# Rows of x by VectorE's 32x32 transposition, gathered in quarters; 8-column logits on TensorE; q's decay on GpSimd; most of w3 loaded behind attention

## The chip, the core and the metric

The kernel runs on one core of a Trainium2 chip, in fp32 and in pairs of fp32r matrices. The metric is the device time of one execution in microseconds (us); lower is better. The engines work in parallel, each from its own instruction stream, and wait for each other on semaphores: TensorE (PE in the profile; its weight loads are PEld), VectorE (DVE), ScalarE (ACT), GpSimd (POOL) and SyncE (SP), which here only starts DMAs.

## The reference

Decayed linear attention feeds a mixture of experts with one expert per token, and that feeds a bilinear network:

```python
# B=4, H=8, S=768, D=64: state (64x64) per head
state = gamma * state + outer(k[t], v[t]);  y[t] = scale * q[t] @ state
x = y, as [3072 tokens, 512]
logits = x @ w_gate + modality_bias[modality_id]        # 8 experts
e = argmax(logits);  gate = softmax(logits)[e]
x = gate * (relu(x @ w1[e]) @ w2[e])                    # w1: 512x1024, w2: 1024x512
out = (((x @ wa) * (x @ wb)) @ w3) @ w_out              # d_ff = 1024
```

## The kernel before

**Attention** runs in 24 units u = 4c + b: six chunks c of 128 tokens, and in each the four batches b. TensorE computes for a unit the scores k q (line 744, into banks 2 and 3), the part that comes from the state (`from_state`, line 762), the part within the chunk (`from_chunk`, line 771) into banks 4 and 5, and the update of the state (`update`, line 783), which the last chunk leaves out. The result is x transposed, features in partitions. ScalarE copies it to `xTu` (four copies, line 553). `rows_and_logits` (line 754) of the unit before then multiplies each of the four 128x128 blocks of `xTu` by `iw`, which is an identity beside the gate weights, so 136 columns: 128 columns give the rows of x, 8 give logits, both in the PSUM pair of banks 6 and 7. VectorE adds up the logits (line 978), ScalarE copies the rows to `x_keep`, and SyncE stores them to `x_rows` in DRAM. VectorE also masks the scores (`prob`, lines 971 and 972), multiplies q by its decay (`qdk`, line 982) and writes the new state (line 990); GpSimd multiplies k by its decay (`kdk`, line 500). SyncE's queue loads q, k (two layouts) and v of a unit, 256 KB each, as soon as the unit four before has updated its state (`s_up`); behind them it stores the rows of five units before and brings in 256 KB of w_out (units 4 to 11) or of w3 (from unit 12 on, two in units 20 to 23). All of x, 24 tiles of 128 tokens, lies in DRAM when attention ends.

**Between attention and the experts** TensorE forms w3 @ w_out in eight products of 24 matmuls each (`w3_product`, line 382). Between them stand the last `rows_and_logits`, `counts` (lines 820 and 821), `token_of_place` (line 884) and, behind the first 6 matmuls of product 7, `first_x` (line 832), which transposes the first gathered window. Meanwhile one long chain of small VectorE operations chooses the experts, sorts the tokens and writes the tables of the windows. `tile_meta` (line 1132) gives GpSimd the list of tokens.

**The experts** run in 8 windows of up to four tiles (in this run 4, 3, 3, 3, 4, 4, 4 and 2 tiles: 512, 384 or 256 columns). `gather` on GpSimd makes the rows of a window with one indirect DMA per tile (line 517, four in a window), 128 rows of 2 KB each, and writes `meta_sorted`. It starts for window w when TensorE has transposed window w-1 (`s_ixp`). TensorE transposes window w+1 in the middle of window w. Its loop over windows has three bodies in the code, for 2, 3 and 4 tiles, in this order; two tests (lines 868 and 870, 871) lead to the right one. SyncE loads the experts' weights, 2 MB for w1 and 2 MB for w2 of each, when the copies in use have been split. The **bilinear part** behind the windows is TensorE's alone and isn't touched.

Of the kernel before, what the change touches and what calls it, by code (L numbers as in the profile page):

```python
# [30 lines left out]
def build(nc, q_t, k_t, k, v, mod_id, w_gate, mod_bias, we1, we2, wa, wb, w3_t, w_out, out):  # L31
# [18 lines left out]
    RANKED = 4  # L50
    XCH = 16
# [19 lines left out]
    def const(name, a):  # L71
# [4 lines left out]
    c_ident = const("c_ident", np.eye(P))  # L76
# [6 lines left out]
                ("token", S * (np.arange(NT) % B) + P * (np.arange(NT) // B) + pos[:, None])]  # L83
# [6 lines left out]
    x_rows = nc.dram_tensor("x_rows", [NT * P, DM], F32).ap()  # L90
# [4 lines left out]
    with ctx:  # L95
# [19 lines left out]
        XW = P + E  # L115
        iw = fixed("iw", [P, KD, XW])
# [3 lines left out]
        tile_meta = fixed("tile_meta", [P, 2, NX])  # L120
        x_id = fixed("x_id", [P, GT], I32)
# [26 lines left out]
        xTu = r("xTu", [P, KD, P])  # L148
# [90 lines left out]
        s_lg = sem("s_lg")  # L239
# [149 lines left out]
        def _(sp):  # L389
# [20 lines left out]
            def x_store(c, b, u):  # L410
                sp.wait_ge(s_keep, u + 1)
                sp.dma_start(x_rows[b * S + c * P:b * S + (c + 1) * P, :], x_keep[:, u, :]).then_inc(s_xst, 16)

            def sp_unit(c, b, u):
# [32 lines left out]
            sp.wait_ge(s_lg, NT)  # L447
# [41 lines left out]
        def _(pool):  # L489
# [13 lines left out]
            each_unit(kdecay)  # L503


            def gather(w):
# [6 lines left out]
                of_window = lambda a: a[:, :, bass.ds(tile, GT)] if w else a[:, :, 0:GT]  # L513
                pool.tensor_copy(x_id[:, :], of_window(tile_meta)[:, 0:1, :].rearrange("p a t -> p (a t)")).then_inc(s_xid, 1)
# [4 lines left out]
                pool.tensor_copy(win_meta[:, :, :], of_window(tile_meta).rearrange("p a t -> p t a")).then_inc(s_wmeta, 1)  # L519
# [17 lines left out]
            pool.tensor_copy(row_id[:, :], meta_in[:, :, 0:1].rearrange("p n a -> p (n a)")).then_inc(s_rowid, 1)  # L537
# [10 lines left out]
        def _(act):  # L548
            act.dma_start(qkv[:, 0, KT, :], slot_v[KT][0, 0, :, :]).then_inc(s_ldq[0], 16)
            act.dma_start(small[:, :], c_small).then_inc(s_const, 16)  # L550
            act.dma_start(iw[:, :, 0:P], c_ident.unsqueeze(1).to_broadcast([P, KD, P])).then_inc(s_gatew, 16)
            act.dma_start(iw[:, :, P:XW], w_gate.rearrange("(c p) e -> p c e", p=P)).then_inc(s_gatew, 16)
            copy = lambda o, i, **kw: act.activation(o, i, ACT.Copy, **kw)  # L553

            def keep(u):

                act.wait_ge(s_lg, u + 1)
                dst = x_keep[:, u, :]
                copy(dst.rearrange("p (j t) -> p j t", j=KD), pair[:, :, 0:P]).then_inc(s_keep, 1)
# [14 lines left out]
            def unit(c, b, u):  # L574

                if u:
                    keep(u - 1)
                act.wait_ge(s_yTu, u + 1)
                for odd in range(2):
                    for r in range(2):  # L580
                        rows = slice((r ^ odd) * D, (r ^ odd) * D + D)
                        i = copy(xTu[rows, odd:KD:2, :], bank[5 - r][rows, :].rearrange("p (j t) -> p j t", j=KD)[:, odd:KD:2, :])
# [12 lines left out]
            keep(NT - 1)  # L595
# [105 lines left out]
            def o_copy(g, t):  # L701
# [4 lines left out]
                w = (meta_in[:, n:n + 1, 1:2] if isinstance(n, int) else meta_in[:, bass.ds(n, 1), 1:2]).rearrange("p a b -> p (a b)")  # L706
# [23 lines left out]
        def _(pe):  # L730
# [16 lines left out]
            def rows_and_logits(u, first):  # L747
                if first:
                    pe.wait_ge(s_gatew, 48)
                pe.wait_ge(s_xTu, u + 1)  # L750
                if not first:
                    pe.wait_ge(s_keep, u)
# [537 lines left out]
```

## Time and profile before

| | us |
|---|---|
| median of 3 runs | 903.19 |
| lowest, highest | 902.89, 903.68 |
| the profiled execution's own time | 903.01 |
| its span, first to last instruction | 901.3 |

A row of the timeline tells when a group of instructions of one engine began and how long it lasted, and in brackets how long the engine had waited for it and for whom. "issue" stands for a wait for nothing that the profile shows. PEclk is the share of full clock granted to TensorE. Durations of TensorE's single instructions overlap; the step from one start to the next is what counts. An fp32 matmul is recorded as two, so eight records stand for four matmuls.

### The profile page before, as it was taken

How to read it: one execution, taken by the hardware profiler on the slowest of the kernel's cores; microseconds unless marked ns; L12 is line 12 of the kernel's file. 1: busy time of each engine (PE TensorE's matmuls, PEld its weight loads, DVE VectorE, ACT ScalarE, POOL GpSimd, SP SyncE). 2: the span in 40 equal slices, each digit the busy share in tenths (PEclk: the TensorE clock that was granted, in tenths of full speed). 3: DMA queues.
4: the chain of work that ended last, by engine and by line, in shares of the span. 5: the costliest groups of instructions: out<-in, count | busy, mean ns of one | idle time of the engine just before them, and what ended most of it. 6: DMA issues, size and time to landing. Idle time of an engine off the chain costs nothing.

```text
span 901.3 us, 13561 instructions
## 1 busy us (share of the span) xinstructions
PE 863.3 (96%) x5236; PEld 739.7 (82%) x5237; DVE 286.2 (32%) x495; ACT 258.8 (29%) x460; POOL 85.5 (9%) x106
## 2 busy tenths in 40 slices
PE   6999999599999999999998999999999999999995
PEld 5888878488999998888888788888888888888884
DVE  2566679531212234121227231121221230230210
ACT  2445533231222233121326222222221221231210
POOL 1222002202020120202000001001001001001001
PEclk9999999889999999999999999999999999999998
DMA  9999751313120343202145102002002002001000
GB/s 326 373 334 363 288 211 47 143 40 103 47 93 0 93 169 110 60 33 55 38 143 184 47 1 82 12 1 82 12 0 81 12 0 93 0 0 47 1 13 35
DMA packets 44006, 84.97 MB, mean 94 GB/s; under 512 B 7744, under 2 KB 8256, under 8 KB 43968
## 3 DMA queue, kind: packets, MB, share of 16 engines
q1 hardware_dynamic: 33376, 60.33, 19.0%
q0 software_dynamic: 4736, 14.72, 5.1%
q10 hardware_dynamic: 5856, 9.40, 3.0%
q8 instruction: 27, 0.44, 0.2%
q14 instruction: 11, 0.09, 0.0%
HBM read 63.42 MB, written 21.00 MB: 94 GB/s over the span
## 4 chain that ended last, share of the span: by engine, by line
PE 91%; DVE 3%; issue 2%; DMA 1%; ACT 1%; ACTq 1%; POOL 0%; DVEq 0%
PE bank L382 79%; PE pair L754 3%; PE bank L771 3%; PE bank L744 2%; PE pair L832 1%; DMA mbias<-n_moe_modality_bias_dram 1%; PE bank L762 1%; PE bank L783 1%; PE bank L884 1%; ACT xTu L553 0%; DVE we_p L953 0%; DVE w3T L953 0%; ACTq L337 0%; DVE prob L971 0%; ACT we_p L553 0%
## 5 line engine op out<-in xcount | busy, mean ns | idle before, releaser
L382 PE MATMUL bank<-yT,wab 128*128 128x512 f32 x1152 | 262.2, 389 | 2.0 <-issue 2.0
L382 PEld LDWEIGHTS bank<-yT,wab 128*128 128x128 f32 x1152 | 216.2, 188 | 47.0 <-issue 2.2
L382 PE MATMUL bank<-xT,we_p 128*128 128x512 f32 (+2 forms) x768 | 153.6, 360 | 13.3 <-issue 10.5
L382 PEld LDWEIGHTS bank<-xT,we_p 128*128 128x128 f32 x768 | 135.4, 191 | 30.9 <-issue 11.8
L382 PE MATMUL bank<-hT,we_p 128*128 128x512 f32 (+2 forms) x768 | 153.6, 357 | 0.0
L382 PEld LDWEIGHTS bank<-hT,we_p 128*128 128x128 f32 x768 | 132.9, 188 | 14.6
L382 PE MATMUL bank<-wc,gT 128*128 128x512 f32 x576 | 131.5, 389 | 0.0
L382 PEld LDWEIGHTS bank<-wc,gT 128*128 128x128 f32 x576 | 108.1, 188 | 22.4
L1232 DVE TENSOR_TENSOR g<-bank,acopy 128x512 f32<-128x512 f32 x48 | 33.2, 692 | 259.1 <-PE bank L382 259.1
L1193 DVE SCALAR_TENSOR_TENSOR hT<-bank,hT 128x512 fp32r<-128x512 f32 x64 | 44.1, 691 | 172.4 <-ACT hT L632 172.4
L632 ACT ACTIVATE hT<-bank 128x512 fp32r<-128x512 f32 x64 | 38.2, 598 | 114.9 <-PE bank L382 114.9
L553 ACT ACTIVATE gT<-g 128x512 fp32r<-128x512 f32 x48 | 30.3, 632 | 136.6 <-DVE g L1232 136.6
L541 POOL DMA_INDIRECT out_dram<-otile,row_id x24 | 23.3, 971 | 378.1 <-ACT otile L553 378.1
L553 ACT ACTIVATE yout<-bank 128x512 f32<-128x512 f32 x32 | 19.1, 597 | 114.6 <-PE bank L382 89.8
L553 ACT ACTIVATE acopy<-bank 128x512 f32<-128x512 f32 x48 | 28.7, 598 | 67.6 <-PE bank L382 67.6
L382 PE MATMUL bank<-w_out_p,w3T 128*128 128x512 f32 x192 | 45.9, 394 | 1.2 <-DVE w3T L953 1.1
L553 ACT ACTIVATE otile<-bank,meta_in 128x512 f32<-128x512 f32 x24 | 16.6, 690 | 100.0 <-PE bank L382 100.0
L953 DVE TENSOR_TENSOR gT<-g,gT 128x512 fp32r<-128x512 f32 x48 | 33.2, 693 | 33.9 <-ACT gT L553 33.9
L382 PEld LDWEIGHTS bank<-w_out_p,w3T 128*128 128x128 f32 x192 | 35.5, 188 | 9.8 <-DVE wc L1022 1.3
L553 ACT ACTIVATE xTu<-bank 64x256 f32<-64x256 f32 x96 | 33.7, 375 | 23.6 <-PE bank L771 23.1
L953 DVE TENSOR_TENSOR xT<-pair,xT 128x512 fp32r<-128x512 f32 x30 | 19.3, 685 | 54.1 <-ACT xT L553 53.9
L754 PE MATMUL pair<-iw,xTu 128*128 128x136 f32 x192 | 29.6, 299 | 4.1 <-DMA mbias<-n_moe_modality_bias_dram 2.8
(144 smaller groups left out, 545.3 us busy)
## 6 DMA issues: line engine op xcount, KB each, us to landing
we_raw<-in_moe_w_dram SPq DMA_DIRECT2D x6, 2048.0 KB, 9.2
yT_sorted<-yout ACTq DMA_DIRECT2D x8, 1024.0 KB, 4.4
qkv<-in_q_t_dram SPq DMA_DIRECT2D x24, 256.0 KB, 3.9
qkv<-in_v_dram SPq DMA_DIRECT2D x24, 256.0 KB, 5.5
x_rows<-x_keep SPq DMA_DIRECT2D x24, 256.0 KB, 5.5
ytile<-yT_sorted SPq DMA_DIRECT2D x6, 1024.0 KB, 5.0
qkv<-in_k_t_dram SPq DMA_DIRECT2D x23, 256.0 KB, 5.3
qkv<-in_k_dram SPq DMA_DIRECT2D x20, 256.0 KB, 5.9
```

The costliest lines, as they stand in the source:

```text
L382: i = pe.matmul(out_, left(a), right(b), start=(first and n == 0), stop=(last and n == 2), **kw)
L541: pool.indirect_dma_start(out[:, :], bass.IndirectOffsetOnAxis(ap=row_id[:, n:n + 1], axis=0), otile[:, n % 2, :], None).then_inc(s_out[n ...
L553: copy = lambda o, i, **kw: act.activation(o, i, ACT.Copy, **kw)
L632: act.activation(hT[:, HI, f, :], bank[f % 2][:, :], ACT.Relu).then_inc(s_hhi, 1)
L744: i = pe.matmul(bank[2 + r][:, t], qkv[head_rows(r), b, KT, t], qkv[head_rows(r), b, QT, t], start=True, stop=True)
L754: i = pe.matmul(pair[:, j, 0:XW], xTu[:, j, :], iw[:, j, :], start=True, stop=True, skip_group_check=True)
L762: pe.matmul(bank[5 - r][out_rows(j, r), j * P:(j + 1) * P], state[head_rows(r), b, j, :], qdk[head_rows(r), b % 2, j, :], start=(j < 2), s ...
L771: i = pe.matmul(bank[5 - r][out_rows(j, r), j * P:(j + 1) * P], qkv[:, b, V, h * D:(h + 1) * D], prob[:, r, j, :], start=(first and j < 2) ...
L783: i = pe.matmul(bank[b % 2][head_rows(r), at:at + D], kdk[:, b % 2, h, :], qkv[:, b, V, h * D:(h + 1) * D], start=(first and b < 2 and j = ...
L953: tt(pair(LO), raw, pair(HI).bitcast(F32), ALU.subtract).then_inc(sm_, 1)
L1193: dve.scalar_tensor_tensor(hT[:, LO, f, :], bank[f % 2][:, :], 0.0, hT[:, HI, f, :].bitcast(F32), ALU.max, ALU.subtract).then_inc(s_hlo, 1)
L1232: tt(g32[:, f % 2, :], bank[2 + f % 2][:, :], acopy[:, f % 2, :], ALU.mult).then_inc(s_g, 1)
```

## The change

It does this:

- TensorE multiplies `xTu` only by the gate weights (`gate_logits`): 8 columns instead of 136. The logits of all units gather in bank 6.
- The rows of x are made by VectorE (`keep`): one 32x32 transposition of `xTu`, now two buffers, into `x_keep`. It transposes inside each group of 32 partitions, so that partition 32a+i holds features of group a of tokens i, 32+i, 64+i and 96+i. ScalarE's copy of the rows and VectorE's sum of logits are gone.
- A token's row therefore lies in DRAM in four pieces of 512 bytes (`x_parts`). `gather` takes one indirect DMA for each piece of each tile: 16 in a window. `tile_id` holds the numbers of the pieces, and six small VectorE operations get the token's number back from the piece's.
- q's decay moves from VectorE to GpSimd.
- The update of the state and VectorE's `new_state` move behind the scores of the next unit.
- w3's pieces 4 to 15 are loaded behind the loads of attention and ahead of the last five stores of rows.
- The experts' loop tests for 4 tiles first.
- The identity of `iw` is no longer loaded; the experts' w1 is laid out by the host in the new order of features.

```diff
...
+    x_parts = nc.dram_tensor("x_parts", [NT * P * QR, P], F32).ap()
...
-                if B + KF <= u < C * B:
+                if B + KF <= u < 2 * B + KF:
                     w3_load(u - B - KF)
-                    if c == C - 1:
-                        w3_load(u - B - KF + B)
             each_unit(sp_unit)
+            for n in range(B, 2 * KF):
+                w3_load(n)
             for u in range(NT - LAG, NT - 1):
                 x_store(u // B, u % B, u)
...
+            def qdecay(c, b, u):
+                pool.wait_ge(s_ldq[b], 32 * (c + 1))
+                pool.wait_ge(s_yTu, u - 1)
+                pool.tensor_tensor(qdk[:, b % 2, :, :], qkv[:, b, QT, :].rearrange("p (j t) -> p j t", j=HP),
+                                   qdect[:, :, :], ALU.mult).then_inc(s_qdk, 1)
...
                 for t in range(GT):
-                    pool.indirect_dma_start(xin[:, t, :], None, x_rows[:, :],
-                                            bass.IndirectOffsetOnAxis(ap=x_id[:, t:t + 1], axis=0)).then_inc(s_xin, 16)
+                    for q in range(QR):
+                        pool.indirect_dma_start(xin[:, t, q * P:(q + 1) * P], None, x_parts[:, :],
+                                                bass.IndirectOffsetOnAxis(ap=x_id[:, t:t + 1, q:q + 1].rearrange("p a b -> p (a b)"), axis=0)).then_inc(s_xin, 16)
...
-            act.dma_start(iw[:, :, 0:P], c_ident.unsqueeze(1).to_broadcast([P, KD, P])).then_inc(s_gatew, 16)
...
                 for j in range(KD):
-                    i = pe.matmul(pair[:, j, 0:XW], xTu[:, j, :], iw[:, j, :], start=True, stop=True, skip_group_check=True)
+                    i = pe.matmul(bank[6][:, u * E:(u + 1) * E], xTu[:, u % 2, j, :], w_gate_t[:, j, :], start=(u == 0 and j == 0), stop=(j == KD - 1),
+                                  skip_group_check=True)
                 i.then_inc(s_xl, 1)
...
                 scores(c, b, u, u == 0)
+                if 0 < u <= NT - B:
+                    update((b - 1) % B, u - 1, u <= B)
                 if u:
-                    rows_and_logits(u - 1, u == 1)
+                    pe.wait_ge(s_xTu, u)
                 if c:
                     from_state(b, u)
+                if u:
+                    gate_logits(u - 1)
                 from_chunk(c, b, u, c == 0)
-                if c < C - 1:
-                    update(b, u, c == 0)
...
-                with pe.If(size < 3):
-                    wide(2)
-                with pe.If(size > 2):
-                    with pe.If(size < 4):
+                with pe.If(size > 3):
+                    wide(4)
+                with pe.If(size < 4):
+                    with pe.If(size > 2):
                         wide(3)
-                    with pe.If(size > 3):
-                        wide(4)
+                    with pe.If(size < 3):
+                        wide(2)
...
+            def keep(u):
+                dve.wait_ge(s_xTu, u + 1)
+                dve.transpose(x_keep[:, u, :].rearrange("p (q j f) -> p q j f", q=QR, j=KD),
+                              xTu[:, u % 2, :, :].rearrange("p j (q t) -> p q j t", q=QR)).then_inc(s_keep, 1)
...
-            dve.tensor_copy(tile_meta[:, :, :].rearrange("p a x -> p (a x)"), bank[0][:, 0:2 * NX]).then_inc(s_tmeta, 1)
+            tt(tile_id[:, :, :], bank[1][:, 0:NX].unsqueeze(2).to_broadcast(wide_q), sm["quarter"].unsqueeze(1).to_broadcast(wide_q), ALU.add).then_inc(s_tmeta, 1)
```

What stands in a row on TensorE in one unit of attention (chunks 1 to 4) is, before, scores, rows with logits, state, chunk, update:

```order
L744 MATMUL bank<-qkv 128x128 x8
L754 MATMUL pair<-iw,xTu 128x136 x4
L762 MATMUL bank<-qdk,state 64x128 x8
L771 MATMUL bank<-prob,qkv 64x128 x8
L783 MATMUL bank<-qkv,kdk 64x64 x8
```

and, after, scores, the update of the unit before, state, logits (8 columns), chunk:

```order
L757 MATMUL bank<-qkv 128x128 x8
L795 MATMUL bank<-qkv,kdk 64x64 x8
L774 MATMUL bank<-qdk,state 64x128 x8
L765 MATMUL pair<-w_gate_t,xTu 128x8 x4
L783 MATMUL bank<-prob,qkv 64x128 x8
```

The update has moved ahead of the state's part, and the 136 columns have become 8.

On GpSimd, at the end of attention and through the first gather (the two DMAs of `meta_sorted` are one write), stands before:

```order
L500 TENSOR_TENSOR kdk<-qkv,small 128x512 x20
L514 CAST x_id<-tile_meta 128x4
L517 DMA xin<-x_rows,x_id 128x512 x4
L519 COPY win_meta<-tile_meta 128x8
L522 DMA meta_sorted<-win_meta 128x4x2
L528 TENSOR_LOAD num_tab
```

and after:

```order
L511 TENSOR_TENSOR qdk<-qkv,qdect 128x512 x4
L532 COPY x_id<-tile_id 128x16
L536 DMA xin<-x_parts,x_id 128x128 x16
L540 COPY win_meta<-tile_meta 128x8
L543 DMA meta_sorted<-win_meta 128x4x2
L549 TENSOR_LOAD num_tab
```

Four products of q stand at the end of attention, and the gather has 16 indirect DMAs where it had four.

On TensorE, from the first test in the loop over windows to the first matmuls behind it, stands before:

```order
L868 COMPARE_AND_BRANCH
L337 ISA
L337 TENSOR_LOAD win_tab
L337 ISA x2
L836 ISA
L839 ISA
L840 ISA
L382 MATMUL bank<-xT,we_p 128x256 x3
```

and after:

```order
L881 COMPARE_AND_BRANCH
L340 ISA
L340 TENSOR_LOAD win_tab
L340 ISA x2
L849 ISA
L852 ISA
L853 ISA
L385 MATMUL bank<-xT,we_p 128x512 x3
```

Behind the first test came the body for 256 columns; now it is the one for 512, so that a window of four tiles is reached without a taken jump, and is left by one over the two other bodies.

## Rows read from the trace of the kernel before

**Rows 1.** Page, part 1: busy time, share of the span, instructions.

```profile
PE 863.3 (96%) x5236; PEld 739.7 (82%) x5237; DVE 286.2 (32%) x495; ACT 258.8 (29%) x460; POOL 85.5 (9%) x106
```

**Rows 2.** By stretch: start:end, length, busy per engine, PEclk, DMA share, GB/s.

```profile
51.90:103.65 51.75, 51.75 (x850) 45.14 (x848) 33.88 (x68) 28.31 (x68) 9.52 (x10) 1.00 1.01 359
170.55:180.34 9.79, 0.00 (x1) 0.01 (x1) 0.69 (x1) 0.60 (x1) 2.21 (x4) 0.75 0.60 239
172.00:174.00 2.00, 0.00 (x0) 0.00 (x0) 0.00 (x0) 0.00 (x0) 1.07 (x3) 1.00 1.02 414
```

**Rows 3.** Timeline, TensorE, one unit of attention: start, us, line, out<-in, count, idle.

```profile
89.92 1.16 PE L744 MATMUL bank<-qkv 64*128 64x128 f32 x16
91.06 1.19 PE L754 MATMUL pair<-iw,xTu 128*128 128x136 f32 x8
92.19 0.67 PE L762 MATMUL bank<-qdk,state 64*64 64x128 f32 x16
92.79 1.09 PE L771 MATMUL bank<-prob,qkv 128*64 128x128 f32 x16
93.71 0.64 PE L783 MATMUL bank<-qkv,kdk 128*64 128x64 f32 x16
94.28 1.16 PE L744 MATMUL bank<-qkv 64*128 64x128 f32 x16
```

**Rows 4.** Timeline, TensorE, a unit without state update.

```profile
106.86 1.16 PE L744 MATMUL bank<-qkv 64*128 64x128 f32 x16
108.47 1.19 PE L754 MATMUL pair<-iw,xTu 128*128 128x136 f32 x8 [0.44 <-ACT xTu L553]
```

**Rows 5.** Timeline, TensorE, start-up and unit 8.

```profile
15.06 2.18 PE L754 MATMUL pair<-iw,xTu 128*128 128x136 f32 x8 [2.76 <-DMA mbias<-n_moe_modality_bias_dram]
...
27.50 1.16 PE L744 MATMUL bank<-qkv 64*128 64x128 f32 x16
...
49.27 1.09 PE L771 MATMUL bank<-prob,qkv 128*64 128x128 f32 x16 [1.44 <-DVE prob L972]
```

**Rows 6.** Groups of instructions by form, TensorE: count | busy us, mean ns | idle.

```profile
L884 PE MATMUL bank<-in_tile,in_lane 128*128 128x72 f32 x48 | 5.5, 274 | 0.0
```

**Rows 7.** The same by form, VectorE and GpSimd, up to 140 us.

```profile
L990 DVE TENSOR_TENSOR state<-bank,small 128x256 f32<-128x256 f32 x20 | 8.5, 424 | 23.1 <-PE bank L783 23.1
...
L1029 DVE TENSOR_REDUCE tmax<-logits 128x24 f32<-128x192 f32 x1 | 0.6, 620 | 0.0
...
L500 POOL TENSOR_TENSOR kdk<-qkv,small 128x512 f32<-128x512 f32 x20 | 20.9, 1043 | 69.4 <-PE bank L783 53.9 <-DMA qkv<-in_k_dram 15.4
```

**Rows 8.** Timeline, TensorE, behind attention and in the windows.

```profile
115.57 1.66 PE L382 MATMUL bank<-w_out_p,w3T 128*128 128x512 f32 x6
...
164.53 1.03 PE L832 MATMUL bank<-small,xin 128*128 128x128 f32 x8
...
180.34 24.53 PE L382 MATMUL bank<-xT,we_p 128*128 128x512 f32 x96 [9.79 <-issue]
...
254.95 8.60 PE L382 MATMUL bank<-hT,we_p 128*128 128x384 f32 x48
...
284.49 1.04 PE L832 MATMUL pair<-small,xin 128*128 128x128 f32 x8
...
334.92 22.07 PE L382 MATMUL bank<-xT,we_p 128*128 128x512 f32 x96 [0.44 <-issue]
```

**Rows 9.** Timeline, GpSimd, the gather of window 0, first and last DMA.

```profile
148.96 1.16 POOL L517 DMA_INDIRECT xin<-x_rows,x_id  x1 [0.29 <-POOL x_id L514]
...
152.95 1.19 POOL L517 DMA_INDIRECT xin<-x_rows,x_id  x1 [0.30 <-issue]
```

**Rows 10.** DMA, 148 to 162 us in 40 slices of 0.35 us: GB/s.

```profile
GB/s 0 0 0 0 0 0 0 0 222 269 211 129 129 257 246 129 105 293 222 105 187 222 234 44 3 0 0 0 0 0 0 0 0 0 0 0 0 0 0 0
```

**Rows 11.** Branches of TensorE's sequencer by line: duration ns min/median/max.

```profile
L868 PEldq COMPARE_BRANCH  x8: 78/214/7007, 168.5 to 468.4; - x8
...
L871 PEldq COMPARE_BRANCH  x7: 68/204/3342, 175.7 to 423.5; - x7
```

More of the change, by code:

```diff
@@ L50, in build @@
     RANKED = 4
+    SQ = 32
+    QR = P // SQ
     XCH = 16
@@ L147, in build @@
         qdect = r("qdect", [P, HP, P])
-        xTu = r("xTu", [P, KD, P])
+        xTu = r("xTu", [P, 2, KD, P])
         x_keep = region(at_i)("x_keep", [P, NT, DM])
@@ L574, in unit @@
             def unit(c, b, u):
-                if u:
-                    keep(u - 1)
                 act.wait_ge(s_yTu, u + 1)
+                if u >= 2:
+                    act.wait_ge(s_keep, u - 1)
                 for odd in range(2):
@@ L581, in unit @@
                         rows = slice((r ^ odd) * D, (r ^ odd) * D + D)
-                        i = copy(xTu[rows, odd:KD:2, :], bank[5 - r][rows, :].rearrange("p (j t) -> p j t", j=KD)[:, odd:KD:2, :])
+                        i = copy(xTu[rows, u % 2, odd:KD:2, :], bank[5 - r][rows, :].rearrange("p (j t) -> p j t", j=KD)[:, odd:KD:2, :])
                 i.then_inc(s_xTu, 1)
@@ L817, in counts @@
                 pe.wait_ge(s_one, 1)
-                pe.wait_ge(s_keep, NT)
                 chosen = onehot[:, :, :].rearrange("p e n -> p (e n)")
-                pe.matmul(bank[6][:, 0:E * NT], sm["before"], chosen, start=True, stop=True)
-                pe.matmul(bank[7][:, 0:E * NT], sm["ones"], chosen, start=True, stop=True).then_inc(s_cnt, 1)
-            w3_product(0, {2: lambda: rows_and_logits(NT - 1, False)})
+                pe.matmul(bank[7][:, 0:E * NT], sm["before"], chosen, start=True, stop=True)
+                pe.matmul(bank[0][:, 0:E * NT], sm["ones"], chosen, start=True, stop=True).then_inc(s_cnt, 1)
+            w3_product(0, {2: lambda: gate_logits(NT - 1)})
             def x_rows(w, chunks):
-                pe.wait_ge(s_xin, w * (16 * GT) + 16 * GT)
+                pe.wait_ge(s_xin, w * (16 * GT * QR) + 16 * GT * QR)
                 for k in chunks:
@@ L1015, in _ @@
             each_unit(unit)
-            keep_logits(NT - 1)
-            dve.wait_ge(s_lg, NT)
+            keep(NT - 1)
+            dve.wait_ge(s_xl, NT)
             def wc_lo(f):
@@ L1027, in _ @@
             over_n = lambda a: a.unsqueeze(2).to_broadcast([P, E, NT])
-            link(tt(logits[:, :, :], logits[:, :, :], bias[:, :, :], ALU.add))
+            link(tt(logits[:, :, :], bank[6][:, 0:NT * E].rearrange("p (n e) -> p e n", n=NT), bias[:, :, :], ALU.add))
             link(dve.tensor_reduce(tmax[:, :], by_n(logits), AX.X, ALU.max))
@@ L1044, in _ @@
             dve.wait_ge(s_cnt, 1)
[L1045 removed]
+            tiles = bank[0][:, 0:E * NT].rearrange("p (e n) -> p e n", e=E)
             flat = lambda a: a[:, :, :].rearrange("p e n -> p (e n)")
[L1047 removed]
+            link(dve.tensor_tensor_scan(flat(cumt), sm["segment"], bank[0][:, 0:E * NT], 0.0, ALU.mult, ALU.add))
             row = lambda i: e_sc[:, i, :]
```

98 lines of the change are left out of this document (48 added, 50 removed).

## The prediction

> **What bounds the kernel now.** TensorE does. The page's first part has it busy for 863.3 of 901.3 us [rows 1], so the reader first looks where it works on something that can be shortened, and where it doesn't work. The table by stretch gives both: in the steady part of attention it is never idle, and between 170.55 and 180.34 us it does nothing for 9.79 us [rows 2]. The timeline of TensorE then tells what a unit of attention is made of [rows 3, 4], what the start looks like [rows 5] and what stands around the stop [rows 8].
>
> A unit starts every 94.28 - 89.92 = 4.36 us. By the steps from start to start it is 1.14 scores, 1.13 rows with logits, 0.60 state, 0.92 chunk, 0.57 update [rows 3]. No engine is waited for in these units. In the last three, without an update, the same 4.35 us hold a wait of 0.44 for `xTu` [rows 4]. DMA is nearly full beside it: share 1.01, 359 GB/s [rows 2].
>
> The stop has its cause in the branches. Line 868 took 7.0 us once and line 871 3.3 us once, while their medians are 0.2 [rows 11]: the two tests that lead to the body for four tiles, for the first time. In the same stretch DMA moved 414 GB/s [rows 2], so whatever code had to be fetched stood behind a load of weights. It costs twice: the clock granted in the stretch falls to a mean of 0.75 [rows 2], so that half of the stretch was at its lower level of 1.2 GHz, and the first 96 matmuls of window 0 take 24.53 us where those of window 4 take 22.07 [rows 8], 2.46 more.
>
> **The change, part by part.**
>
> *Logits.* Four matmuls per unit remain, with full 128x128 weights, but with 8 columns. No row has 8 columns. The nearest has 72 with the same weights: 5.5 us for 48 records, 0.114 each, or 0.91 us for the eight of a unit [rows 6]. From the other side, a line through 72 columns (0.114) and 136 columns (1.13 / 8 = 0.141 [rows 3]) gives 0.087 at 8 columns, 0.70 us for a unit. I take 0.90, next to the measured row, since both rows already lie well above the time of their columns and the weights' part doesn't shrink: 0.22 off each unit (0.42 at the other end). The Trainium skill, "TensorE: Matmul & The Clock Gate", section "LDWEIGHTS (loading the stationary operand)", says that loading weights takes their number of columns divided by 1.2, in ns: 107 for 128 columns. By it eight loads take an estimated 0.86 us, and the sum would be 1 us better over attention; the row of 0.114 agrees with it.
>
> *VectorE in a unit.* It loses q's decay (the form of a 128x512 product) and the sum of logits, and gains the transposition. For that there is no row. A state's product of 256 elements takes 0.424 and a strided reduction of 192 elements 0.620 [rows 7], at most 0.620 / 192 = 3.2 ns an element. So 512 elements take at least 0.42, at a plain rate some 0.7 (two masks of 512 fit into TensorE's 1.13 + 0.60 between scores and chunk [rows 3], under 0.87 each), and at the strided rate 1.65 us. Even with 1.65, two masks of 0.7, a state and a split of 0.7 make 1.65 + 1.4 + 0.42 + 0.7 = 4.17 in a unit, about the new period. I take 0.7, since the transposition reads and writes whole runs of 32: hidden under TensorE.
>
> *GpSimd in a unit.* 20 products of k took 1.043 each [rows 7]; a second one makes 2.1 us in 4.1. q's product waits for the chunk two units before, and nobody but `from_state` of its own unit waits for it, a unit later: hidden. k's product queued behind it waits for the update, now 1.7 us into the next unit, and is needed one unit on: hidden.
>
> *Order.* The update between scores and state fills the time until `xTu` arrives, 1.61 us behind the scores' start [rows 4]: 1.14 + 0.57 = 1.71 covers it. SyncE's loads start 1.7 us later in a unit, three units ahead of their use (12 us): hidden. The wait of 0.44 in the last three units stays, so these fall by 0.22 too. VectorE's biases, which made TensorE wait 1.44 us in unit 8 [rows 5], no longer stand behind an update at a unit's end: I take 0.7 off.
>
> *DMA.* A unit of 1.573 MB (six transfers of 256 KB) in 4.13 us needs 381 GB/s; 414 has been seen [rows 2]. Moving w3 frees units 16 to 23; for units 5 to 15 nothing is freed.
>
> *Start.* TensorE waited 2.76 us for the biases' DMA, issued behind the identity, and then ran its first groups slowly (2.18 us for eight records that take 1.17 later) [rows 3, 5]. Without 256 KB ahead, most of it goes; units 1 to 3 also get 0.2 to 0.5 shorter; loads of units 2 and 3 come next. I take 4.5 us off at unit 4 (27.50 before [rows 5]), between 1.5 and 5.5.
>
> Sum of attention: 4.5 + 17 x 0.22 + 0.7 + 3 x 0.22 = 9.6 us. It ended at 115.57 [rows 8], and will at about 106.0.
>
> *The first gather.* Count from attention's end. The list of tokens reaches GpSimd's first indirect DMA 148.96 - 115.57 = 33.4 us later [rows 8, 9]; the chain starts 0.4 us earlier and has a longer first operation, so 33.2. A step from one indirect DMA to the next is (152.95 - 148.96) / 3 = 1.33 [rows 9]; each still names 128 rows, of 512 bytes where they had 2 KB, so I keep 1.33: a share that goes with the bytes would make it less, and C bounds it from above. Sixteen end at 33.2 + 15 x 1.33 + 1.2 = 54.4. The old ones had landed 2.5 us behind the last (traffic ends at 156.5 [rows 9, 10]); the 2 MB load of the next expert now runs at the same time, for which I add 2: 58.9. TensorE gets there at 164.53 - 115.57 = 49.0 [rows 8]. So a **new wait of 10 us** arises, where four DMAs were hidden.
>
> *The jumps.* They vanish for window 0. Behind the gather come its transposes and 18 matmuls, up to the stop 170.55 - 164.53 = 6.0 us, and about 2.2 for the half clock that the new wait brings as the old stop did. Window 0 starts at 58.9 + 8.2 = 67.1. Before it was at 180.34 - 115.57 = 64.8, plus 2.46 inside the window: 67.2. Gain 0.1. But the body for four tiles now ends in a far jump to code never yet fetched, where it used to run on: between 0 (TensorE has work queued) and 3.3 us [rows 11]. I take 1.7. The six small VectorE operations, at most 0.42 each by the nearest row [rows 7], delay the tables by up to 2.5 us, which the new wait covers; without it they would cost as much.
>
> *Other windows.* 16 x 1.33 + 3 = 24.3 us of gather must fit between the transposes of two windows. The shortest gap is 284.49 - 254.95 = 29.5 us [rows 8]: it fits.
>
> Sum: 903.0 - 9.6 - 0.1 + 1.7 = **895.0 us**, made against the profiled execution's 903.01, which is 0.2 under the median.
>
> **Rivals.**
>
> *A, weights overlap* (15%): a unit's logits cost 0.70 or less. Then 20 units gain 0.2 more, except as DMA limits units 5 to 15. With a gather that lands undisturbed (2 less) this gives 889. For it: the slope between 72 and 136 columns. Against: no fp32 row lies under 0.11.
>
> *B, DMA caps attention* (10%): if it gives no more than now, units 5 to 15 stay at 4.36 and 11 x 0.22 is lost; with a start that gains 1.5 the time is 900.5. For it: share 1.01 [rows 2]. Against: 414 GB/s.
>
> *C, GpSimd bounds the windows* (7%, slower): if an indirect DMA of quarters takes longer than the old, at 2.3 us a step, the first gather ends 15 us later, and each of the three gaps of some 29.5 us is exceeded by 16 x 2.3 + 3 - 29.5 = 10: 45 more, 940. The windows begin to wait from 1.66 us a step, and the kernel is slower than before from 1.71, where 15 x 0.38 in the first gather and 3 x 16 x 0.05 in the windows eat the 8 us gained. For it: nothing shows a gather of quarters. Against: the steps of the old form lie at 1.33 [rows 9].
>
> *D, every far jump stalls* (5%): each window of four tiles leaves by a jump; if code didn't stay, the other three would pay 1.7 too, 900.1. The Trainium skill, "Runtime: NRT & Kernel Launch", section "Instruction fetch mechanics", says that a taken branch outside the present two pages forces a fetch. Here later windows pass line 868 in 0.2 us [rows 11]: fetched code stays, and the trace speaks against it.
>
> **How the numbers follow.** Forecast 895 with 63%; its own range 890.5 to 899 comes from the start (3 up, 1 down), the logits (up to 4 down), contention and jump (2 each way). The range 887 to 901.5 leaves out C and the rest of A. Within 0.2% (1.8 us, about what a measurement tells from no change) falls 3%, faster 90%, slower 7%.
>
> **What would show it.** In the profile after: logits of 0.9 a unit and a period near 4.13; attention's end near 106; 16 indirect DMAs 1.33 apart; TensorE waiting 7 to 11 us for `xin` before its first transposes, and no stop behind product 7. If that wait is missing, the gather is cheaper than I think and the time is near 887; if waits for `xin` show in later windows, C holds.

## The result and the profile after

| | us |
|---|---|
| changed kernel, median of 4 runs | 983.78 (982.37 to 984.67) |
| kernel before, beside it, median of 4 runs | 903.04 (901.95 to 903.68) |
| ratio, 95% interval | 1.0894 (1.0875 to 1.0913) |
| the profiled execution, its span | 982.37, 980.2 |

The change makes the kernel 8.9% slower, where 0.9% faster was forecast. The page of the changed kernel, part 1 and the groups of part 5 that changed most (line, engine, names, count | busy us, mean ns | idle before them, who ended it):

```profile
PE 881.8 (90%) x5236; PEld 754.2 (77%) x5237; DVE 285.5 (29%) x481; ACT 244.5 (25%) x436; POOL 202.1 (21%) x222
...
L385 PE MATMUL bank<-xT,we_p 128*128 128x512 f32 (+2 forms) x768 | 172.9, 389 | 71.0 <-DVE hT L1206 55.6
...
L536 POOL DMA_INDIRECT xin<-x_parts,x_id x128 | 122.1, 954 | 40.3 <-issue 36.6
```

The same two rows of the page before, and of the changed kernel with four indirect DMAs per gather (`a_4dma`, below):

```profile
L382 PE MATMUL bank<-xT,we_p 128*128 128x512 f32 (+2 forms) x768 | 153.6, 360 | 13.3 <-issue 10.5 <-DVE hT L1193 2.8
```

```profile
L385 PE MATMUL bank<-xT,we_p 128*128 128x512 f32 (+2 forms) x768 | 155.3, 364 | 11.7 <-issue 8.4 <-DVE hT L1204 2.4 <-DVEq L1236 0.9
```

TensorE's busy share fell from 96% [rows 1] to 90%. The first products of the experts lost 71.0 - 13.3 = 57.7 us to idle time and were busy for 19.3 us more; from window 0 to the bilinear part the granted clock had a mean of 0.91, where it was 0.99. Attention did get shorter. The timeline of TensorE, first the start and a steady unit of attention, then what answers [rows 8]:

```profile
14.57 1.16 PE L757 MATMUL bank<-qkv 64*128 64x128 f32 x16
...
22.01 1.16 PE L757 MATMUL bank<-qkv 64*128 64x128 f32 x16
...
86.76 1.16 PE L757 MATMUL bank<-qkv 64*128 64x128 f32 x16
87.85 0.69 PE L795 MATMUL bank<-qkv,kdk 128*64 128x64 f32 x16
88.47 0.67 PE L774 MATMUL bank<-qdk,state 64*64 64x128 f32 x16
89.06 1.06 PE L765 MATMUL pair<-w_gate_t,xTu 128*128 128x8 f32 x8
90.05 1.09 PE L783 MATMUL bank<-prob,qkv 128*64 128x128 f32 x16
91.08 1.16 PE L757 MATMUL bank<-qkv 64*128 64x128 f32 x16
...
108.04 1.20 PE L385 MATMUL bank<-w_out_p,w3T 128*128 128x512 f32 x4
...
163.39 1.97 PE L845 MATMUL bank<-small,xin 128*128 128x128 f32 x8 [5.04 <-DMA xin<-x_parts,x_id]
...
172.85 8.66 PE L385 MATMUL bank<-xT,we_p 128*128 128x512 f32 x36 [0.93 <-DVEq L1238]
189.80 16.71 PE L385 MATMUL bank<-xT,we_p 128*128 128x512 f32 x60 [8.30 <-issue]
...
232.84 6.00 PE L385 MATMUL bank<-xT,we_p 128*128 128x384 f32 x24 [2.75 <-issue]
244.17 6.10 PE L385 MATMUL bank<-xT,we_p 128*128 128x384 f32 x26 [5.34 <-DVE hT L1206]
...
343.25 15.62 PE L385 MATMUL bank<-xT,we_p 128*128 128x384 f32 x72 [12.06 <-DVE hT L1206]
393.89 18.16 PE L385 MATMUL bank<-xT,we_p 128*128 128x512 f32 x72 [11.12 <-DVE hT L1206]
...
577.87 2.31 PE L385 MATMUL bank<-yT,wab 128*128 128x512 f32 x9 [1.73 <-issue]
```

Attention ends at 108.04 (115.57 before), window 0 starts at 172.85 (180.34), so up to here 7.5 us are gained. From there to the bilinear part it is 577.87 - 172.85 = 405.0 us, where it was 499.86 - 180.34 = 319.5: **85.5 us are lost inside the windows**. Each window but the last has a new stop of 5 to 12 us behind its first matmuls. TensorE waits there for `hT`, the activated first product, which VectorE makes out of ScalarE's copy.

Why is `hT` late? Window 3, all engines (columns as above; the sixteen indirect DMAs of the gather for window 4 stand 1.25 us apart):

```profile
318.11 8.59 PE L385 MATMUL bank<-hT,we_p 128*128 128x384 f32 x48
...
319.21 0.98 POOL L536 DMA_INDIRECT xin<-x_parts,x_id  x1 [0.48 <-POOL x_id L532]
...
322.57 0.60 ACT L573 ACTIVATE yout<-bank 128x512 f32<-128x512 f32 x1 [3.48 <-PE bank L385]
...
326.75 0.94 POOL L536 DMA_INDIRECT xin<-x_parts,x_id  x1 [0.30 <-issue]
...
326.76 4.43 PE L385 MATMUL bank<-xT,we_p 128*128 128x384 f32 x24
...
333.36 0.60 ACT L573 ACTIVATE yout<-bank 128x512 f32<-128x512 f32 x1 [10.19 <-remote]
...
338.01 0.94 POOL L536 DMA_INDIRECT xin<-x_parts,x_id  x1 [0.30 <-issue]
...
341.88 1.31 ACT L645 ACTIVATE hT<-bank 128x512 fp32r<-128x512 f32 x2 [7.92 <-remote]
342.51 1.52 DVE L1206 SCALAR_TENSOR_TENSOR hT<-bank,hT 128x512 fp32r<-128x512 f32 x2 [22.58 <-ACT hT L645]
```

TensorE's 48 records end at 318.11 + 8.59 = 326.70. ScalarE, which waits for nothing else, takes their result at 333.36, 6.7 us later, while the result of the group before was taken at once (322.57). The two groups of `xT` products that ended by 331.2 are taken at 341.88. The profile names no releaser ("remote"), and VectorE and ScalarE have nothing else to do. So TensorE's semaphore signals arrive late: the trace has the two semaphores' updates at 333.34 and 341.86, 0.02 us ahead of ScalarE's starts. The last comes 2.9 us behind the end of the gather's last indirect DMA (338.01 + 0.94). By its records TensorE itself was done and had gone on with the next group. The table by stretch for 186 to 190 us, inside window 0's stop (busy us of PE, PEld, DVE, ACT, POOL; PEclk; DMA share; GB/s), shows it idle and at its lower clock level, 1.2 GHz:

```profile
186.00:190.00 4.00, 0.20 (x1) 0.20 (x2) 0.69 (x1) 1.38 (x2) 2.39 (x4) 0.50 0.14 41
```

Below, a signal's **delay** is the time from the end of TensorE's group in the timeline to the start of ScalarE's copy of it, and "at +7.5" means 7.5 us behind the start of a gather's first DMA. In the profile of before every delay around the gathers is 0.04 us. The Trainium skill, "Perfetto Trace Analysis", section "Tensor Engine Instruction (MATMUL, LD_WEIGHTS)", says that TensorE's end in a profile is computed, and that its semaphore update becomes visible only in a later step, for which it gives no duration; here that step took 0.04 us or up to 15.

Where the trace lets one look, other engines' signals aren't held. TensorE's signal of 154.34 was held until 163.96, but VectorE's for `w3T`, of 156.59, let TensorE's next weight load begin at 156.71. ScalarE's copy of `hT` that ended at 177.71, inside the second gather, was taken by VectorE at 177.74.

### The profile page after: what moved, and what is told of

Same layout as the page of the kernel before. It is cut to its first block, busy times and chain, and to the rows that moved or that the text cites. A ratio compares the mean times of both kernels' runs of the same rounds, so it can differ in the third digit from the quotient of the medians.

```text
span 980.2 us, 13660 instructions
## 1 busy us (share of the span) xinstructions
PE 881.8 (90%) x5236; PEld 754.2 (77%) x5237; DVE 285.5 (29%) x481; ACT 244.5 (25%) x436; POOL 202.1 (21%) x222
## 3 DMA queue, kind: packets, MB, share of 16 engines
q1 hardware_dynamic: 33376, 60.33, 17.6%
## 4 chain that ended last, share of the span: by engine, by line
PE 78%; another core or an unknown queue 9%; issue 4%; DVE 4%; POOL 2%; ACT 1%; ACTq 1%; DMA 1%; DVEq 0%
PE bank L385 66%; PE bank L783 3%; PE bank L757 3%; PE pair L765 2%; POOL xin L536 2%; PE pair L845 1%; PE bank L795 1%; PE bank L774 1%; DVE w3T L966 1%; ACTq L340 0%; DVE hT L1206 0%; DMA qkv<-in_q_t_dram 0%; ACT hT L645 0%; DVE in_lane L1093 0%
## 5 line engine op out<-in xcount | busy, mean ns | idle before, releaser
L385 PE MATMUL bank<-xT,we_p 128*128 128x512 f32 (+2 forms) x768 | 172.9, 389 | 71.0 <-DVE hT L1206 55.6
L385 PEld LDWEIGHTS bank<-xT,we_p 128*128 128x128 f32 x768 | 150.5, 212 | 93.0 <-DVE hT L1206 58.4
L536 POOL DMA_INDIRECT xin<-x_parts,x_id x128 | 122.1, 954 | 40.3 <-issue 36.6
L1245 DVE TENSOR_TENSOR g<-bank,acopy 128x512 f32<-128x512 f32 x48 | 33.2, 692 | 258.8 <-PE bank L385 258.8
L385 PEld LDWEIGHTS bank<-w_out_p,w3T 128*128 128x128 f32 x192 | 36.2, 192 | 11.2 <-issue 3.0
L573 ACT ACTIVATE otile<-bank,meta_in 128x512 f32<-128x512 f32 x24 | 16.5, 690 | 100.0 <-PE bank L385 100.0
```

Of the source, the lines that this page charges most:

```text
L385: i = pe.matmul(out_, left(a), right(b), start=(first and n == 0), stop=(last and n == 2), **kw)
L536: pool.indirect_dma_start(xin[:, t, q * P:(q + 1) * P], None, x_parts[:, :], bass.IndirectOffsetOnAxis(ap=x_id[:, t:t + 1, q:q + 1].rearra ...
L1245: tt(g32[:, f % 2, :], bank[2 + f % 2][:, :], acopy[:, f % 2, :], ALU.mult).then_inc(s_g, 1)
```

## The experiments

Names with b_ start from the kernel before, names with a_ from the changed one. The code shown is shortened, and words in place of an expression stand for a view of the tensor. Every time stands beside runs of the kernel before on the same chip (903.4 to 905.3 us).

**Is it the gather?** `b_quarters` puts nothing but the gather of sixteen into the kernel before:

```diff
 for t in range(GT):
-    pool.indirect_dma_start(xin[:, t, :], None, x_rows[:, :], x_id[:, t])
+    for q in range(4):
+        pool.indirect_dma_start(xin[:, t, q * P:(q + 1) * P], None, x_rows as pieces of 128, x_id[:, q, t])
```

> The kernel before, with its gather alone changed to sixteen indirect DMAs of 128 pieces of 512 bytes (four small VectorE operations make the numbers of the pieces). Theory N (a long row of indirect DMAs on GpSimd holds back TensorE's signals, whatever their size) and theory S (pieces of 512 bytes do it) both expect the new stops behind the first 24 matmuls of every window and some 85 us for them, the difference between 405.0 us from window 0 to the bilinear part in the changed kernel and 319.5 before, plus about 12 for the later first gather: 990 to 1005 us. Theory O (another part of the change does it) expects only the first gather's delay: about 915 us, with every window of experts as long as before.

Measured 996.05 us (995.00 and 997.11), ratio 1.102. The gather alone does it, more than the whole change. The first late signal of windows 1 to 6 was delayed by 6.8 to 12.7 us. Theory O fell.

`a_4dma` is the changed kernel without it:

```diff
 for t in range(GT):
-    for q in range(QR):
-        pool.indirect_dma_start(xin[:, t, q * P:(q + 1) * P], None, x_parts[:, :], x_id[:, t, q])
+    pool.indirect_dma_start(xin[:, t, :], None, x_parts as rows of 512, x_id[:, t])
```

> The changed kernel with four indirect DMAs of 128 rows of 2 KB in a gather, as before (they read whole rows of the buffer of pieces, so the experts get other numbers of the same size). Theories N and S: no stops in the windows; attention as in the changed kernel (ends at 108.0, 7.5 us ahead of before), the stop of 9.8 us and the half clock behind it (2.5) gone, 3.8 us for the jump out of window 0: about 903 - 7.5 - 12.3 + 3.8 = 887 us. Theory O: the stops stay, 970 us or more.

Measured 897.02 (896.77 to 898.45), ratio 0.9929 (0.9904 to 0.9954). No signal is late. From window 0 to the bilinear part it takes 493.64 - 165.50 = 328.1 us against 405.0: **the late signals cost 76.9 us**. It is 10 us above what I expected. Some 7 of them are in the jumps, for which I had put 3.8:

```profile
165.50 22.05 PE L385 MATMUL bank<-xT,we_p 128*128 128x512 f32 x96 [0.93 <-DVEq L1236]
...
214.18 18.50 PE L385 MATMUL bank<-xT,we_p 128*128 128x384 f32 x96 [3.08 <-issue]
256.07 18.27 PE L385 MATMUL bank<-xT,we_p 128*128 128x384 f32 x96 [4.98 <-issue]
293.09 16.91 PE L385 MATMUL bank<-xT,we_p 128*128 128x384 f32 x96 [0.32 <-issue]
```

**What do the jumps give?** `b_order` changes only the order of the bodies, as in the diff ahead of the prediction.

> The kernel before with only the order of the three window bodies changed (four tiles first). Theory P (the prediction): the stop of 9.79 us ahead of window 0 and the 2.46 us of half clock inside it go, one far jump of 1.7 us comes: about 892.5 us. Theory F: the code of the other bodies is missed later instead, as in a_4dma, where 3.08 us of idle stand ahead of window 1 and 4.98 ahead of window 2, and these windows' first 96 matmuls took 18.50 and 18.27 us instead of 16.91: 11.0 back, about 902 us.

Measured 904.17 (901.90 to 905.72), ratio 1.0006 (0.9994 to 1.0019): nothing. The stop of 9.79 us is gone; in its place stand 2.88 and 4.92 us ahead of windows 1 and 2, and window 2's first 96 matmuls take 19.76 us. Presumably the code behind window 0's body and behind the first run of the next body is now what has to be fetched; no row names it.

**Which property of the gather?** `b_rows32` has sixteen DMAs, but the rows of 2 KB and the bytes of before; each reads `x_id[0:32]` and writes 32 partitions.

> The kernel before, with sixteen indirect DMAs in a gather that bring 32 rows of 2 KB each: as many DMAs as in the changed kernel, but the bytes and the pieces of the kernel before (each reads the first 32 tokens of its tile, so the experts compute other rows). Theory N: the stops come as in the changed kernel, 980 to 1005 us. Theory S: no stops; the first gather is late by at most 12 x 1.3 = 16 us, of which some is hidden: 903 to 915 us.

Measured 1001.5 (998.73 and 1004.26). The size of the pieces is not it, and theory S fell. Here TensorE itself stumbles too, once two of its signals are held up, those of 242.91 and 245.01 (timeline, window 1):

```profile
246.95 0.34 PE L382 MATMUL bank<-xT,we_p 128*128 128x384 f32 x1 [0.72 <-issue]
249.08 0.34 PE L382 MATMUL bank<-xT,we_p 128*128 128x384 f32 x1 [1.79 <-issue]
251.88 0.48 PE L382 MATMUL bank<-xT,we_p 128*128 128x384 f32 x1 [2.46 <-issue]
```

`b_busy` keeps GpSimd at work without DMAs:

```diff
+for i in range(30):
+    pool.tensor_tensor(idle[:, 1, :], idle[:, 0, :], idle[:, 0, :], ALU.add)   # each waits for the last
```

> The kernel before; behind the four indirect DMAs of each gather GpSimd computes 30 sums of 128x192 elements that nobody uses (some 14 to 20 us), so it is occupied as long as in a gather of sixteen DMAs, without issuing any. Theory D (it is the issuing of DMAs by GpSimd that holds back TensorE's signals): no signal is late, 903 to 906 us. Theory B (any long stretch of work on GpSimd does): signals of TensorE that fall over 7.5 us behind a gather's start come late and the time is 960 to 1000 us.

Measured 908.63 (908.39 to 909.37), every delay 0.04. The sums took 17.44 us. The 5 us lost lie ahead of window 0 (186.57 instead of 180.34), where TensorE waits 3.83 us for VectorE's `w3T` instead of 0.91, not inside the windows. Theory B fell.

`b_plain16` issues twelve plain DMAs from GpSimd behind the four indirect ones.

> The kernel before; behind the four indirect DMAs of each gather GpSimd issues twelve plain DMAs of 128 pieces of 64 bytes that nobody uses. Theory D1 (any DMA issued by GpSimd counts): signals are held as in b_rows32, 980 to 1005 us. Theory D2 (only the indirect form does): no signal is late, 903 to 908 us.

Measured 904.88 (902.47 to 906.98), every delay 0.04. The twelve took 6.45 us to issue, a row of DMAs of 11.2 us in all, into which TensorE's signals at +7.5 fall. The runs speak for D2: plain DMAs, at least of this small size, don't count.

**Number, time or pace?** `a_pause` adds a wait behind every four of the sixteen:

```diff
         pool.indirect_dma_start(...)
+    pool.wait_ge(s_xin, w * (16 * GT * QR) + 16 * QR * (t + 1))
```

> The changed kernel; GpSimd waits behind every four of its sixteen indirect DMAs until they have landed. Theory R (an unbroken row of more than some 7 us of issuing is what holds the signals): no signal is late; a gather takes 4 x (5.0 + 2.2) = 29 us, 9 more than now, which delays window 0 by 9 and is just covered in the other windows: 983.8 - 85 + 9 = 908 us, between 900 and 925. Theory Q (sixteen DMAs in a gather do it, with pauses too): 980 us or more.

Measured 911.64 (911.59 and 911.68). With all sixteen DMAs in each gather, no signal is late. ScalarE in window 3, beside the rows above, while the gather ran from 299.77 to 325:

```profile
307.30 0.60 ACT L574 ACTIVATE yout<-bank 128x512 f32<-128x512 f32 x1 [3.56 <-PE bank L385]
...
309.80 0.60 ACT L646 ACTIVATE hT<-bank 128x512 fp32r<-128x512 f32 x1 [1.91 <-PE bank L385]
311.88 0.60 ACT L646 ACTIVATE hT<-bank 128x512 fp32r<-128x512 f32 x1 [1.48 <-PE bank L385]
```

`b_rows64` has eight DMAs of 64 rows in a row, `b_spread` the same with two sums behind each.

> The kernel before, with eight indirect DMAs of 64 rows of 2 KB in a gather, in one row without a pause (both halves of a tile read its first 64 tokens, so the experts compute other rows). Theory K (the seventh indirect DMA of an unbroken row starts the hold): the seventh starts some 7.2 us behind the first, so TensorE's signals at +7.5 and +10 us are late by 2 to 6 us, until the gather ends at about +12, and little is lost by that: 903 to 910 us. Theory L (over eight are needed): no signal is late.

> The same eight indirect DMAs, with two sums of 128x192 elements (0.58 us each) behind each, so that one starts every 2.35 us and the gather takes 19 us without an idle moment on GpSimd. Theory T (time: some 7.5 us of unbroken work with indirect DMAs in it): signals of TensorE from +7.5 us on are late. Theory K (number): only those behind the seventh, from +14.1 us on, are. Theory V (rate: the queue behind an indirect DMA empties in the pauses): none is.

One run each: 915.73 and 913.69 us. In `b_rows64` the signals at +7.5 us are delayed by 4.0 us and those at +10.1 by 1.4, as theory K wants. In `b_spread` none is. ScalarE in the two, around the gather from 259.49 and around the one from 226.65:

```profile
262.86 0.60 ACT L554 ACTIVATE yout<-bank 128x512 f32<-128x512 f32 x1 [3.48 <-PE bank L382]
270.99 0.60 ACT L554 ACTIVATE yout<-bank 128x512 f32<-128x512 f32 x1 [7.53 <-remote]
```

```profile
231.32 0.60 ACT L561 ACTIVATE yout<-bank 128x512 f32<-128x512 f32 x1 [4.78 <-PE bank L384]
236.76 0.60 ACT L561 ACTIVATE yout<-bank 128x512 f32<-128x512 f32 x1 [4.84 <-PE bank L384]
```

So it is the pace: something fills while indirect DMAs follow each other 1.16 to 1.25 us apart, and empties when they come every 2.3 us. T fell, and K holds only at the fast pace: signals that ended 1.09 us behind the sixth DMA's start were on time, those at 1.20 us, as the seventh began, were late. (`a_best6` below shows that a seventh isn't needed.) The 10 to 12 us that both lose stand, in the first, half in stops behind late signals (2.54 and 2.32 us are the longest); in the second all ahead of window 0, which starts at 188.78.

`a_pace` lies between, with one sum of 128x160 elements behind each DMA of the changed kernel.

> The changed kernel with one sum of 128x160 elements (some 0.5 us) behind each indirect DMA, so that one starts every 1.75 us and a gather takes 28 us. In b_spread, at 2.3 us, no signal was late; at 1.17 and 1.25 they were from the seventh DMA on. Theory V1 (what fills up empties at one DMA in less than 1.75 us): no signal is late, and with the first gather 7 us later than in the changed kernel the time is 983.8 - 85 + 7 = 906 us, 903 to 915. Theory V2 (it empties more slowly than that): late signals in the second half of each gather, 920 us or more.

Measured 915.22 (913.86 and 916.59), one DMA every 1.72 us, every delay at most 0.46. V1 holds: the limit lies between 1.25 and 1.72 us.

**What must be in a DMA?** `b_rows8` splits a tile into 8, 8, 8 and 104 rows, `b_rows16` into 16, 16, 16 and 80, `b_rows24` into 24, 24, 24 and 56.

> The kernel before; a tile's 128 rows of 2 KB come in four indirect DMAs of 8, 8, 8 and 104 rows, sixteen in a gather (each begins with the tile's first tokens, so the experts compute other rows). As many DMAs as in the changed kernel, as many rows and bytes as before. Theory N (the number of indirect DMAs that follow each other too fast counts, whatever is in them): TensorE's signals are late from the seventh on, 980 to 1005 us. Theory E (what is in them counts, rows or bytes): hardly any is late, 903 to 925 us.

> As b_rows8, but a tile's 128 rows come in indirect DMAs of 16, 16, 16 and 80 rows: numbers that share out evenly over the 16 DMA engines, as 128, 64 and 32 do and 8 and 104 don't. Theory U (the hold needs DMAs whose completions come from all 16 engines in step, at a pace above one in 1.75 us): signals of TensorE are late from the seventh on, 980 to 1005 us. Theory W (small DMAs among them are enough to end it): no late signals, 905 to 915 us, as b_rows8.

> The same with 24, 24, 24 and 56 rows, which don't share out evenly over 16 engines. Theory U: no late signals, 905 to 915 us. Theory X (DMAs of under 16 rows were what ended the hold in b_rows8): late signals, 980 to 1005 us.

One run each: 911.07, 995.31 and 998.04 us. In `b_rows8` every delay is 0.04, in the others they reach 15 us, though all issue one DMA every 1.15 to 1.3 us with the same rows and bytes. Even shares (U) fell with `b_rows24`, and W with `b_rows16`. It looks as if DMAs of 8 rows didn't count and those of 16 to 128 did alike; in `b_rows8` the larger ones come 4.8 us apart. What in the chip distinguishes them stays open.

**Versions that might be faster.** `a_tokens` puts the pieces together on the way out:

```diff
-sp.dma_start(x_parts[at:at + P * QR, :], x_keep[:, u, :])
+for a in range(QR):
+    sp.dma_start(x_rows[at:at + P, a * P:(a + 1) * P] as (i q f), x_keep[SQ * a:SQ * a + SQ, u, :] as (i q f))
```

> The changed kernel, but the pieces are put in their places on the way out: SyncE stores a unit's x with four DMAs whose elements are 512 bytes, so that a token's 2 KB lie together, and the gather is that of the kernel before. The same as a_4dma if the stores cost nothing, about 887 us. If 512-byte elements take DMA twice the time, 0.26 of the 1.57 MB of a unit cost 17% more: units of 4.3 us would go to at most 5.0 in the eleven units in which DMA is full, 895 us. Theory O: 970 us or more.

Measured 902.74, but from 899.18 to 909.63; ratio 0.9986 (0.9959 to 1.0013). No late signals, but not the 887 to 895 that I had expected. In the profiled execution (909.63) units 1 to 3 took 6.77 us each, with TensorE at half its later pace (2.08 us for scores that take 1.16 later; the profile's record of the clock begins only at 34.3 us), and two later ones waited 1.02 and 0.91 us for k's loads. What the stores in pieces cost by themselves isn't shown.

`a_best4` and `a_best6` pause in all gathers but the first and put the first transposes behind 18 records of product 7.

> The changed kernel with pauses behind every four indirect DMAs (until they have landed) in all gathers but the first, whose TensorE waits for it anyway, and with the first transposes of x behind 18 instead of 6 records of product 7. Against a_pause (911.6): window 0 starts at 172.85 as in the changed kernel instead of 180.84, 8.0 less, and up to 3.5 us of the wait for x (5.04) are filled with matmuls: 900.5 us, between 899 and 905. If signals are held in the first gather to TensorE's cost it stays near 905.

> The same with pauses only ahead of the seventh and the thirteenth indirect DMA. Theory K with the limit at the seventh: no signal is late and the time is that of a_best4 within 1.5 us, 899 to 904. If the limit counts time (7.5 us) or pauses don't reset it wholly, signals at +7.5 and behind are late in some windows: 910 us or more.

Measured 906.46 (ratio 1.0032, 1.0007 to 1.0056) and 908.33 (1.0062, 1.0031 to 1.0093). Window 0 starts at 169.30 and 169.77, but the pauses then make the second gather end behind its use (`a_best4`):

```profile
201.14 1.97 PE L847 MATMUL pair<-small,xin 128*128 128x128 f32 x8 [4.34 <-DMA xin<-x_parts,x_id]
```

I had expected 900.5: the waits for landing are longer (4.1 and 5.5 us) where the experts' 2 MB are loading. In the first gathers, which have no pause, one product's signal is 10.0 and 9.8 us late. Elsewhere groups of four delay two signals, by 0.4 and 0.45 us, and groups of six delay nine by 0.5 to 1.9. In `a_best6`, with the seventh DMA only at 301.98:

```profile
291.89 8.59 PE L385 MATMUL bank<-hT,we_p 128*128 128x384 f32 x48
...
293.00 0.98 POOL L538 DMA_INDIRECT xin<-x_parts,x_id  x1 [0.48 <-POOL x_id L532]
...
299.28 0.95 POOL L538 DMA_INDIRECT xin<-x_parts,x_id  x1 [0.30 <-issue]
...
301.69 0.60 ACT L575 ACTIVATE yout<-bank 128x512 f32<-128x512 f32 x1 [4.73 <-PE bank L385]
```

TensorE's group ended at 300.49, and ScalarE took it 1.2 us later, 8.7 us behind the row's first DMA. Put side by side, the ends of the holds are regular. Counted from the start of a row's first DMA, the last late signal was taken at +5.7 and +5.8 us in rows of four (`a_best4`), at +8.6 to +8.7 in rows of six (once +7.2), at +11.5 in the rows of eight of `b_rows64` (once +10.7), and at +22.5 to +23.1 in rows of sixteen, whether these were issued every 1.16 or every 1.25 us (once +20.5). That is 1.41 to 1.46 us for each DMA of the row. An estimate from these rows: something works through indirect DMAs of 16 or more rows at some 1.4 us each, slower than GpSimd issues them in a row, and TensorE's signals can have to wait until it has caught up. The limit between 1.25 and 1.72 us fits. What it is no run shows.

`b_ident` keeps of the change only what helped the start:

```diff
-act.dma_start(iw[:, :, 0:P], c_ident...).then_inc(s_gatew, 16)
+for j in range(KD):                                  # on GpSimd
+    pool.tensor_copy(iw[:, j, 0:P], sm["ident"]).then_inc(s_iwi, 1)
-pe.wait_ge(s_gatew, 48)
+pe.wait_ge(s_gatew, 16)
+pe.wait_ge(s_iwi, KD)
```

> The kernel before; GpSimd copies the identity of iw from the tables that are loaded anyway (four copies) instead of a DMA of 256 KB, and TensorE's first rows and logits wait for the gate weights but not for the biases. This is the part of the change's start that has nothing to do with the gather. The gate weights landed at 10.05 us in the changed kernel; unit 1's rows and logits can then start at about 12.3 instead of 15.06 and go at full pace: 3 to 4 us less, 900 us, between 898.5 and 902.

Measured **899.05** (898.55 to 899.42), ratio 0.9955 (0.9938 to 0.9972). It beats both kernels (`a_4dma` is lower still, but leaves out the pieces: it reads whole rows of `x_parts`). TensorE at the start; in [rows 5] the rows and logits of unit 1 began at 15.06 and took 2.18, and unit 4 began at 27.50, 3.0 us later than here:

```profile
13.22 1.34 PE L756 MATMUL pair<-iw,xTu 128*128 128x136 f32 x8
...
24.52 1.16 PE L745 MATMUL bank<-qkv 64*128 64x128 f32 x16
```

## Why the prediction was wrong

**The step that failed** is "Other windows": "16 x 1.33 + 3 = 24.3 us of gather must fit between the transposes of two windows ... it fits". It does fit: sixteen steps of 1.25 us and the rest take 22 us, and no window but the first waits for `xin`. The error is the inference that a gather which ends in time costs nothing. Rival C was on the slower side with the right engine, but asked only whether a step takes longer than 1.33; it takes 1.25. The price came in a place where I had no term, TensorE's signals: 76.9 us. The profile of before couldn't show it, since its rows have four indirect DMAs, and none of TensorE's signals ended between +4.7 and +7.4. That a row four times as long had no example there was a reason for a bound, and I gave none.

Point by point:

- **Start**: 4.5 forecast, 27.50 - 22.01 = 5.5 measured, at the top of the range that I gave (1.5 to 5.5).
- **Logits**: 0.90 a unit forecast, 90.05 - 89.06 = 0.99 measured, and the chunk behind them grew from 0.92 to 1.03, which I had no term for. The period is 4.32 instead of 4.13: over 17 units 0.7 us gained, not 3.7. So rival A fell. B fell too: the 4.32 is the same in units 5 to 15, where DMA is nearly full, and behind them, and TensorE waits for nothing in them. The estimate of 0.86 for eight loads, from the Trainium skill, "TensorE: Matmul & The Clock Gate", section "LDWEIGHTS (loading the stationary operand)", was further off than the row of 0.114 a record; 0.124 came.
- **Attention's end**: 106.0 forecast, 108.04 measured. The 1.44 us for the biases is gone, twice what I had put, and the waits of 0.44 stayed, as forecast. That it came within 2 us of the forecast is partly luck: the start and the biases gave more, the logits less.
- **First gather**: it starts 141.24 - 108.04 = 33.2 behind attention's end, as forecast. Its steps have a mean of (160.82 - 141.24) / 15 = 1.31 (1.33 in [rows 9]). It had landed at 163.39, 55.4 behind attention instead of 58.9, and TensorE came later than I thought (it had waited 2.40 ahead of product 7), so the new wait is 5.04 us, not 10. From attention's end to window 0 it is 64.8, where 67.1 was forecast and 64.8 stood before.
- **Jumps**: 9.79 + 2.46 were to go and 1.7 to come back. They went, and 3.08 + 4.98 us and 2.95 of half clock came (`a_4dma`). The far jump out of window 0 was seen, the second one, a window later, wasn't. The Trainium skill, "Runtime: NRT & Kernel Launch", section "Instruction fetch mechanics", has a taken branch outside the present two pages force a fetch; the two stops agree. I had weighed that rule against windows that came later and passed line 868 in 0.2 us, which isn't evidence on the first pass through a body. Rival D fell: in `a_4dma` no window behind the third has such a stop.
- **GpSimd and VectorE in a unit, order**: hidden, as forecast. For the transposition I had taken 0.7 us between 0.42 and 1.65; the groups by form, VectorE, have it at 702 ns:

```profile
L990 DVE STREAM_TRANSPOSE x_keep<-xTu 128x512 f32<-128x512 f32 x24 | 16.8, 702 | 2.1 <-ACT xTu L573 2.1
```


Without the late signals 983.8 - 76.9 = 906.9 us would be left, not 895. Attention gave 7.5 us instead of 9.6, nothing was gained from there to window 0, and the windows without late signals still take 328.1 us where they took 319.5: these 8.6 us are what the jumps moved there, 3.08 + 4.98 + 2.95 - 2.46. `a_4dma`, which has no wait in its first gather, stands at 897.

What stays open: what it is that fills and holds back TensorE's signals, and why eight rows are too few to count. One rival is untested: every time here comes from an execution whose span and clock were recorded, and of the 256 landings of `xin` in a gather the changed kernel's trace has only 41 to 103, where that of `a_pace` has all 256 in every gather of the windows. The kernel before, without a late signal, also misses some of its 64. So whether the hold needs the recording, no run tells.

## What to carry to other kernels

When a change multiplies the number of one kind of instruction, look whether the profile has a row of them as long as the new one. Where it hasn't, bound what the row does to the other engines, also where the issuing engine has time to spare. On this chip keep GpSimd's indirect DMAs to four in a row (at most 0.45 us late here), or space them by 1.7 us or more. And take the cheap part of a change by itself: four copies in place of one DMA at the start, and no wait for the biases, gave the only gain that lasted.

## What the runs showed of the hardware

- Indirect DMAs of 16 or more rows that GpSimd issues 1.15 to 1.3 us apart delay TensorE's semaphore signals, from the seventh on by 1.2 to 15.3 us: of 95 signals whose group ended between the start of the seventh and the end of the last DMA, in the changed kernel, `b_quarters` and `b_rows16` to `b_rows64`, 93 were late. The other two are the first signals of window 0 in `b_quarters` (+16.5 us) and `b_rows24` (+17.6 us), after TensorE had been idle for 8 us.
- The last late signal comes free some 1.4 us times the number of DMAs behind the first one's start: 5.7 us for four, 8.7 for six, 11.5 for eight, 22.5 to 23.1 for sixteen.
- At 1.72 or 2.3 us apart, in groups of four with a wait for landing, with 8 rows in three of four, or in rows of four, no delay above 0.5 us was seen; in groups of six nine signals were 0.5 to 1.9 us late. Twelve plain DMAs and 17 us of sums on GpSimd did nothing to the signals.
- With two signals held up, TensorE went on for a while and then issued single matmuls 2 to 3 us apart (`b_rows32`).
- Eight columns with 128x128 weights in fp32 cost 0.124 us a record, against 0.141 for 136 columns.
